# The second MLP's up products split over two 64-row tiles of TensorE

## The reference

```python
scores = scale * np.matmul(q, k.transpose(0, 1, 3, 2))      # 4 x 8 heads, 576 x 576, depth 64
scores = np.where(scores >= max - tau, scores, -1e9)        # then softmax, then @ v
h = x @ w_in                                                # MLP 1: 2304 x 512 -> 1024
ln = layernorm(h * softmax(h)) * g_ln;  x = ln @ w_out      # 1024 -> 512
h = x @ w_in                                                # MLP 2: 2304 x 512 -> 2048
g = np.maximum(h, 0.0) + np.log1p(np.exp(-np.abs(h)))       # softplus
return g @ w_out                                            # 2048 -> 512
```

## Time and profile before

| | before |
|---|---|
| median of 3 runs | 888.11 us (887.92 to 888.94) |
| the profiled execution | 887.9 us, span 886.2 us |
| granted clock, mean | 0.998 |
| PE busy | 861.7 us (97%) |
| PEld busy | 716.5 us (81%) |
| DVE / ACT / POOL busy | 638.6 / 567.1 / 324.3 us |
| up products (L1152) | 1152 matmuls |
| down products (L1241) | 864 matmuls |

### The profile page before, as it was taken

How to read it: one execution, slowest core, us unless ns; L and a number is a source line. 1 busy time by engine, 2 the same in 40 slices (tenths; PEclk the granted TensorE clock), 3 DMA queues, 4 the chain that set the end, 5 groups by cost and what they waited for, 6 DMA issues and landing times.

```text
span 886.2 us, 16881 instructions
## 1 busy us (share of the span) xinstructions
PE 861.7 (97%) x6248; PEld 716.5 (81%) x6248; DVE 638.6 (72%) x1286; ACT 567.1 (64%) x1040; POOL 324.3 (37%) x425
## 2 busy tenths in 40 slices
PE   6899999999999999999999999999999999999998
PEld 4566666666667889898899999999999999999996
DVE  6899999999955633615447578867858858868865
ACT  3787988787876533424356566666666667667664
POOL 3554677555544601102021232333332232233232
PEclk9999999999999999999999999999999999999999
DMA  6713423343001100000021500000100000000000
GB/s 167 205 47 81 110 55 75 88 108 108 18 1 37 37 1 1 2 1 1 1 84 49 178 1 1 37 0 1 37 1 1 37 1 1 36 0 0 36 0 36
DMA packets 30394, 37.16 MB, mean 42 GB/s; under 512 B 4720, under 2 KB 18544, under 8 KB 30320
## 3 DMA queue, kind: packets, MB, share of 16 engines
q1 hardware_dynamic: 29920, 35.90, 14.7%
q10 hardware_dynamic: 400, 0.30, 0.1%
HBM read 31.46 MB, written 4.72 MB: 41 GB/s over the span
## 4 chain that ended last, share of the span: by engine, by line
PE 55%; issue 25%; POOL 9%; DVE 9%; ACT 0%; DMA 0%; ACTq 0%; POOLq 0%; DVEq 0%
PE h_ps L1040 12%; PE y_ps L1176 11%; POOL w_lo L527 9%; PE m_ps L1152 8%; PE f_ps L1241 7%; DVE ntop L837 7%; PE s_ps L1072 7%; PE o_ps L1112 5%; PE t_ps L1088 2%; PE lt_ps L1188 1%; PE s_ps L1067 1%; DVE kept L853 1%; DVE inv L869 0%; PE l_ps L1083 0%; DMA k_sb<-k_t 0%
## 5 line engine op out<-in xcount | busy, mean ns | idle before, releaser
L1152 PE MATMUL m_ps<-y_hi,w 128*128 128x384 f32 x768 | 211.8, 337 | 0.0
L527 POOL TENSOR_TENSOR w_lo<-w_rest,w_hi 128x512 fp32r<-128x512 f32 x84 | 110.3, 1313 | 253.5 <-ACT w_hi L700 253.4
L1152 PEld LDWEIGHTS m_ps<-y_hi,w 128*128 128x128 f32 x768 | 140.3, 188 | 3.9
L580 ACT ACTIVATE expd<-s_ps,ntop 128x576 f32<-128x576 f32 x144 | 106.2, 741 | 51.6 <-DVE ntop L837 51.6
L1152 PE MATMUL m_ps<-y_lo,w 128*128 128x384 f32 x384 | 129.0, 336 | 0.0
L700 ACT CAST w_hi<-w_rest 128x512 fp32r<-128x512 f32 x84 | 52.2, 622 | 109.1 <-PE f_ps L1241 105.7
L465 POOL TENSOR_SCALAR kept<-kept,inv 128x576 f32<-128x576 f32 x144 | 105.8, 750 | 38.8 <-DVE inv L869 38.7
L837 DVE TENSOR_REDUCE ntop<-s_ps 128x1 f32<-128x576 f32 x144 | 107.4, 757 | 14.3 <-PE s_ps L1072 8.3
L1241 PE MATMUL f_ps<-w_hi,g_hi 128*128 128x512 f32 x288 | 113.4, 394 | 0.7 <-POOL w_lo L527 0.7
L966 DVE SCALAR_TENSOR_TENSOR g<-u,z 128x384 f32<-128x384 f32 x96 | 53.2, 554 | 84.1 <-ACT u L716 84.1
L1241 PE MATMUL f_ps<-w_hi,g_lo 128*128 128x512 f32 x288 | 113.8, 395 | 0.0
(11 more groups left out here) (89 smaller groups left out, 1650.5 us busy)
## 6 DMA issues: line engine op xcount, KB each, us to landing
q_sb<-q_t SPq DMA_DIRECT2D x28, 288.0 KB, 5.2
v_sb<-v_main SPq DMA_DIRECT2D x16, 256.0 KB, 3.2
stage<-w_in SPq DMA_DIRECT2D x16, 256.0 KB, 2.7
out<-o_sb SPq DMA_DIRECT2D x5, 768.0 KB, 3.6
w_rest<-w_out SPq DMA_DIRECT2D x7, 512.0 KB, 5.4
k_sb<-k_t SPq DMA_DIRECT2D x21, 144.0 KB, 4.6
stage<-w_in SPq DMA_DIRECT2D x4, 512.0 KB, 8.1
stage<-w_out SPq DMA_DIRECT2D x4, 512.0 KB, 6.3
```

The lines of the kernel that those rows point to most:

```text
L527: nc.gpsimd.tensor_tensor(w4[1][n % 2], w4_rows(n % F2, 1)[:, 0, :], f32(w4[0][n % 2]), ALU.subtract).then_inc(w4lo_made, 1)
L580: nc.scalar.activation(expd[:, tile % 2, :].rearrange("p (a b) -> p a b", a=2), s_ps[tile % 2][:, :, 0:HALF], ACT.Exp, bias=ntop[:, tile % ...
L1152: last = nc.tensor.matmul(m_ps[n % 4][:, 0:GC], w[n % F2][:, k, :], y[odd][:, k, :], start=(k == 0 and m == 0), stop=(k == C - 1 and m == 2))
```

## The change

`up_pair` takes the place of `up` for items 4 to 95. It treats the items `pair` and `pair + 1` (an even one and the one after it) together. In the even step (phase 0) item `pair` is multiplied with rows 0 to 63 of every 128-deep slice, and item `pair + 1` with rows 64 to 127, in alternation on the two row tiles; in the odd step (phase 1) it is the other way round. So a phase has 24 matmuls (12 pairs) of 64-row weight tiles with 384 columns, and both items' banks are complete only at the end of phase 1, when `m_made` is raised by 2. The down products keep their places: one stands between the two phases. Phase 0 waits for `g1_made` to reach `pair` - 2 (both banks free); phase 1 waits for the new semaphore `m_half`, which phase 0 raised. In the first group the wait on `w_lo` is made once a pair, for the later item's weights.

```diff
+            def up_pair(j, n):
+                pair, phase = j - n % 2, n % 2
+                odd = n // F2
+                if phase == 0:
+
+                    wait(pe, g1_made, pair - 2)
+                else:
+                    pe.wait_ge(m_half, pair - EARLY + 2)
+                for k in range(C):
+                    for m, (w, y) in enumerate(((w3[0], y_hi), (w3[0], y_lo), (w3[1], y_hi))):
+                        for q in range(2):
+                            item = (n - phase + (q ^ phase)) % F2
+                            last = nc.tensor.matmul(m_ps[item % 4][:, 0:GC], w[item][halves[q], k, :],
+                                                    y[odd][halves[q], k, :], start=(phase == 0 and k == 0 and m == 0),
+                                                    stop=(phase == 1 and k == C - 1 and m == 2))
+                if phase == 0:
+                    last.then_inc(m_half, 2)
+                else:
+                    last.then_inc(m_made, 2)
...
             def mlp2(i, n):
                 j = 2 * F2 * i + n
                 if within(j, F2 * MG):
-                    if isinstance(j, int) and j < F2:
-                        if j >= EARLY:
-                            first_up(j)
-                    else:
-                        if n % F2 == 0:
-
-                            pe.wait_ge(ylo_made, 2 * i + n // F2 + 1)
-                        up(j, n)
+                    if isinstance(j, int) and EARLY <= j < F2 and n % 2 == 0:
+
+                        pe.wait_ge(w_lo, parts(C + F1 // 2 + j + 2))
+                    if n % F2 == 0:
+
+                        pe.wait_ge(ylo_made, 2 * i + n // F2 + 1)
+                    if not (isinstance(j, int) and j < EARLY):
+                        up_pair(j, n)
```

More of the change, by code:

```diff
@@ L248, in build @@
         yhi_made, ylo_made = sem("yhi_made"), sem("ylo_made")
+        m_half = sem("m_half")
         m_made, abs_made, z2_made = sem("m_made"), sem("abs_made"), sem("z2_made")
```

## The result

| | before | changed |
|---|---|---|
| median | 888.01 us (885.83 to 888.94, 4 runs) | 925.23 us (923.56 to 926.37, 4 runs) |
| ratio | | 1.0424, 95% interval 1.0401 to 1.0447 |
| profiled execution, span | 887.9, 886.2 us | 926.37, 924.6 us |
| PE busy | 861.7 us (97%) | 899.4 us (97%) |

The account below looks back on a forecast made before the run. TensorE was taken as the bound. Tiling changes of 36.8 us plus 1.6 for the tail, with 0 gained inside phases, gave +38.4 us and a forecast of 926.5 us (chance 0.52), 8-in-10 range 908 to 974.

Parts of the forecast that it names:

- The sum: Whole kernel: 36.8 for tiling changes plus 1.6 for the tail minus 0, +38.4 us; own range 922 to 929.
- The bound: TensorE, busy 97% of the span, sets the time; other engines count only if they become late.
- The row of nines: TensorE's granted clock reads 9 in all 40 slices of the profile, taken as 2.4 GHz throughout.
- Step 1: Inside a phase: 12 pairs side by side at today's 0.174 us a slot, gain 0; other end 15.5 us gained.
- faster slots: Rival, phases: row-tile pairs stream at 0.160 to 0.163 us a slot, same switches, +25, 913 us; chance 0.22.
- Step 2: Between up and down products: 92 round trips to row tiles at 0.40 us, unhidden, 36.8 us.
- Step 3: TensorE's waits on `m_half`, `g1_made` and `w_lo`: all met in time, each 0.
- Step 4: Items reach ACT and VectorE in twos, the even one later: hidden, with over 3 us to spare.
- Step 5: Tail: items 94 and 95 released together, so down(94) starts later, +1.6 us once.
- Weight loads bind: Rival, phases: the two tiles' loads queue at 0.108 us, 46 us more, 973; chance 0.10, shared with a late engine.
- the pairs don't overlap: Rival, phases: matmuls of a pair run one after the other, 192 us more, 1119; chance 0.08.
- Faster than before: Rival: switches between fp32r products cost nothing and slots fall to 0.160 us, 874 us; chance 0.05.

Follow-up runs that it names:

- experiment 3: The changed kernel's order, waits and release in twos, with each up product again 12 full-array matmuls: 890.47 us, ratio 1.0032 to the kernel before.
- experiment 1: The changed kernel with down products on the two row tiles too, so tiling does not change between items 4 and 95: 893.83 us, ratio 1.0071.
- experiment 5: The changed kernel with only one of the two row tiles used in each phase, half of every up product left out: 925.66 us, ratio 1.0432.
- Experiment 10: The kernel before with the whole second MLP split into bf16 high and low parts instead of fp32r ones: 859.22 us, ratio 0.9695.
- experiment 4: The kernel before with one extra 64-row matmul on one row tile between up and down products of items 4 to 95: 937.53 us, ratio 1.0561.
- 4b: The kernel before with one extra 128-row, full-array matmul between up and down products of items 4 to 95: 902.46 us, ratio 1.0176.
- Experiment 2: The changed kernel with both phases of a pair back to back, then both down products: 928.07 us, ratio 1.0458 to the kernel before.
- experiment 7: The changed kernel with the second MLP's steps written out on TensorE, without the loop of 32 steps: 924.45 us, ratio 1.0417.

## Why the prediction was right, point by point

**The sum.** +38.4 was forecast, and the two spans differ by 38.5. That the figures are so close is luck; the medians differ by 37.2. The changes of tiling came out about 2 us cheaper than the 36.8 and the tail 0.2 cheaper than the 1.6, and 1.3 at the loop's return and 1.1 ahead of the change, none of which the sum had, filled the gap. One slip is in the sum's own range: trips of 0.41 give 92 x 0.41 + 1.6 + 888.1 = 927.4 and not 929.

**The bound.** Right. TensorE stayed at 97%, and no engine came late in the steady part (experiment 3: 376.00 of 376 us busy). The row of nines was read too strongly, though: a slice is 22 us long, and 3.4 us at half clock, from 29.0 on in the attention phase, lie within one of them. In the second MLP the clock held up to the tail.

**Step 1, the arithmetic of a phase.** Right: gain 0. I chose the nearest row in kind, the fp32r stream at 0.174, over the split tiles' 0.160 (by single starts, 119.58 and 119.74, it is 0.163). Experiments 1 and 5 show that a tile's stream keeps that pace alone or in a pair, which settles "faster slots" (913). The argument against that rival was that its rows stream each column twice and would hide a limit on feeding. Experiment 10 shows that the excess goes with the operands' width; that feeding is the limit, and that those rows stream twice, no run shows.

**Step 2, the tiling's change.** Right in mechanism and close in size: 0.381 for 0.40 in the isolated pair 4 and 4b, 35.1 us for 36.8. The term's parts, from the profile after: about 0.09, 0.11, 0.09 and 0.10 against 0.095, 0.10, 0.095 and 0.105. The price read from 16 transposes between two other products carried over to half-row products of another type, and experiment 4 shows the same price with a single matmul inside. The tiling page's sentence (the Trainium skill, TensorEngine Tiling (Array Packing), Key Properties: changing the mode drains TensorE) agrees with the 0.09 on the way in and the 0.09 on the way out. The other half of the price, the first load behind each drain, is read from the trace alone.

**Step 3, PE's new waits.** Right where the change has them: `m_half` costs nothing with a down product between. Experiment 2 gives the price when the cover is gone, 0.34 us.

**Step 4, items in twos.** Right, hidden; experiment 3.

**Step 5, the tail.** Idle 2.14 where about 2.3 was forecast: 1.4 for 1.6. Missing from the step: after such an idle the granted clock fell in four profiled executions (experiments 1, 3, 5 and 7), which cost another 1.4 us in experiment 3, and did not in two (the changed kernel, experiment 2).

**Not in the sum.** 1.3 us at the loop's return; the slightly smaller trips (0.381 for 0.40, 1.7 us less) outweigh it.

**The rivals.** "Weight loads bind" and "the pairs don't overlap": no; two loads in 0.18, and the two starts of a pair mostly 4 ns apart. "Faster than before" needed a round trip under 0.15 us. The rule that stood beside it (the Trainium skill, TensorE: Matmul & The Clock Gate, The mechanism: a load runs under a matmul only in another row group, though the same section also names a background weight buffer as a way ahead) disagrees with this case a second time: in experiment 1, as in the kernel before, loads of 0.18 us on the rows of the running matmul are hidden, with up products 0.174 apart.

## What to carry to other kernels

Splitting a contraction that already fills the array over two row tiles gained nothing here, and each excursion to another tiling cost about 0.38 us with 128-column 4-byte weights: two drains and two first loads that nothing covers. Price it from any place in the trace where the tiling already changes, by the distance of starts across it; a busy share will not show it. And when matmuls run a constant few per cent over their column count, look at the width of what they read before reordering them.

## What the runs showed of the hardware

- At 2.4 GHz fp32r operands stream at 0.174 us for 384 columns and 0.231 for 512, contiguous bf16 at 0.1625 and 0.216, bf16 read from every second half-word at about 0.171 (384 columns). At 1.2 GHz 512 fp32r columns took 0.427. A pair of fp32 products of 192 columns on two column tiles took 0.163, by the starts at 119.58 and 119.74 in the trace before.
- DVE slows beside POOL. In the changed kernel 43 of 89 casts on DVE (L981) overlap POOL's L528, after 20 of 89 before, and both stretch: these casts take 1.34 us on average and the other 46 take 0.36, and POOL's subtraction takes 1.67 where it was 1.31 on average before. Over 410 us of the changed kernel the cast's mean is 832 ns, over 376 us before it 528:

```profile
L981 DVE CAST g_hi<-g 128x384 fp32r<-128x384 f32 x89 | 74.0, 832 | 3.1
```

```profile
L980 DVE CAST g_hi<-g 128x384 fp32r<-128x384 f32 x89 | 47.0, 528 | 3.1
```

  Here it is hidden behind TensorE (DVE busy 675.4 us for 638.6).
- TensorE's granted clock was on its lower level for 3.4 us after or at the end of an idle of 2.12 to 2.31 us in the tail in four profiled executions, and stayed up in two with idles of 2.14 and 2.48.
- TensorE's loop of 32 steps stalled at its return in two kernels: 1.3 us with 33 matmuls a step and 2.8 with 42. With 21 it did not, and neither did experiment 2's loop, with 33 a step in another order; the cause is open.
